# The taps' tile made 16 columns narrower: every tile allocated behind it moves down by 64 bytes

## The reference

```python
# 1: each head (8 heads of 24 channels) mixes 7 tokens with softmaxed taps, causal, zero-padded
w = softmax(weight, axis=-1)                      # weight: 8 x 7
out[b, s, h] = sum_k w[h, k] * x_pad[b, s + k, h]
# 2: a gated feed-forward, 192 -> 1536 -> 192
g = x @ w_gate;  x = (g * sigmoid(g) * (x @ w_val)) @ w_out
# 3: a second one with ELU, 192 -> 2048 -> 192
h = x @ w_in;  y = where(h > 0, h, exp(min(h, 0)) - 1) @ w_out2
```

## Time and profile before

| | us |
|---|---|
| median of 3 runs | 1193.2 (1192.63 to 1193.23) |
| the profiled execution's own time | 1191.55 |
| its span, first to last instruction | 1189.7 |
| PE busy | 1184.1 (100%) |
| PEld busy | 1051.1 (88%) |
| DVE, ACT, POOL busy | 772.7, 664.6, 699.6 |

### The profile page before, as it was taken

The page is one execution under the profiler, slowest core; times in us unless marked ns, Lnnn a source line. Parts: engine busy times, 40 slices in busy tenths (PEclk is TensorE's granted clock), DMA queues, the critical chain, the costliest instruction groups (busy, mean ns, idle before and its releaser), DMA issues.

```text
span 1189.7 us, 31406 instructions
## 1 busy us (share of the span) xinstructions
PE 1184.1 (100%) x11804; PEld 1051.1 (88%) x11804; DVE 772.7 (65%) x1192; ACT 664.6 (56%) x1113; POOL 699.6 (59%) x517
## 2 busy tenths in 40 slices
PE   9999999999999999999999999999999999999998
PEld 8889889898898988989888898888989889898898
DVE  7877565675656766566665766647667475675665
ACT  6557455464654646546465564655646555465564
POOL 6378565474654746547465474654756556475565
PEclk9999999999999999999999999999999999999999
DMA  8512011121101211012110021100212002120110
GB/s 179 121 43 45 18 31 32 31 44 31 24 20 31 44 31 26 18 31 44 31 35 17 22 44 31 35 18 22 44 31 44 9 22 44 31 44 9 32 33 15
DMA packets 103957, 43.38 MB, mean 36 GB/s; under 512 B 75889, under 2 KB 93937, under 8 KB 103921
## 3 DMA queue, kind: packets, MB, share of 16 engines
q1 hardware_dynamic: 103104, 42.29, 16.5%
q10 hardware_dynamic: 816, 0.59, 0.2%
HBM read 16.12 MB, written 6.29 MB: 19 GB/s over the span
## 4 chain that ended last, share of the span: by engine, by line
PE 97%; DVE 2%; issue 1%; ACT 0%; DMA 0%; SPq 0%; DVEq 0%; ACTq 0%
PE up L897 54%; PE down L897 42%; DVE hid_lo L740 1%; DVE mixed L702 1%; DVE hidden L759 0%; DMA in_b_lo<-in_b_lo 0%; DVE x_t L720 0%; DVE in_b_lo L708 0%; ACT act L568 0%; PE down L1108 0%; ACT out_w L324 0%; ACT hidden L641 0%; ACT in_b_hi L526 0%; ACT in_a_hi L646 0%; SPq L370 0%
## 5 line engine op out<-in xcount | busy, mean ns | idle before, releaser
L448 POOL TENSOR_TENSOR hid_lo<-hidden,hid_hi 128x512 fp32r<-128x512 f32 x435 | 607.1, 1407 | 464.6 <-ACT hid_hi L585 302.2
L897 PE MATMUL down<-out_w,hid_hi 64*128 64x384 f32 x2040 | 300.8, 355 | 0.0
L759 DVE TENSOR_TENSOR hidden<-act,up 128x512 f32<-128x512 f32 x191 | 131.0, 686 | 242.4 <-ACT act L568 242.4
L897 PE MATMUL down<-out_w,hid_lo 64*128 64x192 f32 x2040 | 263.0, 247 | 0.0
L800 DVE TENSOR_SCALAR act<-up 128x512 f32<-128x512 f32 x256 | 164.8, 686 | 107.5 <-PE up L897 105.4
L897 PE MATMUL up<-in_b_hi,up_w_hi 64*128 64x512 f32 x1128 | 226.1, 391 | 0.2 <-DMA in_b_lo<-in_b_lo 0.2
L897 PE MATMUL up<-in_b_lo,up_w_hi 64*128 64x512 f32 x1128 | 225.2, 389 | 0.0
L897 PE MATMUL up<-in_b_hi,up_w_lo 64*128 64x512 f32 x1128 | 224.5, 388 | 0.0
L585 ACT ACTIVATE hid_hi<-hidden 128x512 fp32r<-128x512 f32 x192 | 121.5, 633 | 174.9 <-DVE hidden L759 156.5
L621 ACT ACTIVATE hid_hi<-hidden 128x512 fp32r<-128x512 f32 x256 | 156.7, 628 | 96.8 <-DVE hidden L816 79.9
L897 PEld LDWEIGHTS down<-out_w,hid_lo 64*128 64x128 f32 x2040 | 202.1, 187 | 4.5
(11 more groups left out here) (99 smaller groups left out, 1100.6 us busy)
## 6 DMA issues: line engine op xcount, KB each, us to landing
x_raw<-x_dram SPq DMA_DIRECT2D x136, 64.0 KB, 2.3
out_dram<-stage SPq DMA_DIRECT2D x15, 384.0 KB, 2.7
in_b_hi<-in_b_hi SPq DMA_DIRECT2D x32, 128.0 KB, 2.3
in_b_lo<-in_b_lo SPq DMA_DIRECT2D x32, 128.0 KB, 2.3
swapped<-halves SPq DMA_DIRECT2D x32, 128.0 KB, 2.3
in_a_hi<-in_a_hi SPq DMA_DIRECT2D x30, 128.0 KB, 2.3
in_a_lo<-in_a_lo SPq DMA_DIRECT2D x30, 128.0 KB, 2.3
stage<-w_out_dram SPq DMA_DIRECT2D x7, 384.0 KB, 4.4
```

The costliest lines, as they stand in the source:

```text
L448: return pool.tensor_tensor(hid_lo[:, slot, :], hidden[:, s, :], hid_hi[:, slot, :].bitcast(F32), ALU.subtract)
L759: v.tensor_tensor(hidden[:, f % 2, :], act[:, f % 2, :], val_bank(f, n)[:, :], ALU.mult)\
L897: return nc.tensor.matmul(dst, lhsT, rhs, start=start, stop=stop, skip_group_check=True)
```

## The change

One constant, `WIDE`, goes from 120 to 104.

```diff
@@ mix_ffn_ffn
     WARM_BEFORE, WARM_AFTER = 6, 2
     PAIRS = (TAPS + 1) // 2
-    WIDE = 120
+    WIDE = 104
     assert N1 % RING == 0 and N2 % RING == 0 and 2 * TAIL == P and PER_BATCH == 8 and CHUNKS == 16
```

## The result

The changed kernel takes **1182.1 us** (median of 5 runs, 1180.6 to 1182.9) against 1193.2 (5 runs): ratio 0.9906, 95% interval 0.9893 to 0.992. It is faster by 11 us. The forecast was no change, in a range of 1187 to 1210, so both the forecast and the range were wrong.

A forecast was written before the change was run, and what follows sets the result against it. PE was taken as the bound, pair count times distance. Only the taps term counted, all others 0: 1191.55 - 0.1 = 1191.45 us for the profiled execution, 1193.2 - 0.1 = 1193.1 us against the median, range 1187 to 1210.

The forecast's parts named there:

- What bounds the kernel: In the chunks nobody makes PE wait; time is the number of matmul pairs times their distance, 228.8 ns for 512 columns.
- The columns, and what is on top of them: A 512- or 384-column pair costs its columns, 213 or 160 ns, plus about 15.5 ns.
- the 15.5 ns on top: Part of a 512-column pair's 228.8 ns beyond its columns, the only part a place in memory can change.
- The 192-column pairs: In down2_pair, each truly costs some 0.11 us, the length of one weight load, and delays its follower.
- the debt: About 0.025 us each 192-column pair hands on, because its follower's weights are not loaded when it has streamed.
- The taps matmuls, -0.1 us: At the start, 16 of 120 columns less in two fp32 matmuls saves between nothing and 0.14 us; taken as -0.1.
- DVE, ACT, POOL and DMA, 0: Their tiles move from 192 to 128 modulo 256; no effect, bounded by 0.5 us for engines, 0.2 us for DMA.
- The operands' places, 0: Moving and loaded operands all at 128 modulo 256 cost 4856 pairs nothing, nor 1016 that run on their load.
- case 3: Last project pair ahead of a down2_pair, moving tile and loading weights both at 192: 0.23 us, indistinguishable from other pairs.
- Case 4: Last 192-column pair of a down2_pair, moving tile and loading weights both at 128: 0.34 us with follower, as elsewhere.
- The faster rival: Reads in the same place run together, so 15.5 ns falls towards 3: 1132 us at full effect; chance 0.18.
- The slower rival: Equal places make a shared resource worse: values from 1196 to 1222 us, most below 1210; chance 0.24.

The follow-up runs named there:

- number 1: Changed kernel plus 64 unused bytes behind the taps' tile, putting all later tiles back at 192 modulo 256: 1193.0 us, ratio 1.0006.
- number 2: Changed kernel with the taps' tile 120 columns wide again and 192 unused bytes behind it, later tiles at 128 modulo 256: 1181.6 us, ratio 0.9904.
- number 3: Changed kernel plus 64 unused bytes ahead of the first weights, so weights and moving tiles all lie at 192 modulo 256: 1181.5 us, ratio 0.9908.
- experiment 8: Changed kernel with all tiles that TensorE does not read in the chunks put back to 192 modulo 256: 1182.4 us, ratio 0.991.
- Experiment 12: Changed kernel with only up1_w_lo and up2_w_lo at 192 modulo 256, everything else at 128: 1198.2 us, ratio 1.0041.
- number 7: Changed kernel with only hid_hi and hid_lo put back to 192 modulo 256: 1191.7 us, ratio 0.9986.
- experiment 16: Changed kernel with both operands of project at 192 modulo 256 and both of down1 and down2_pair at 128: 1191.9 us, ratio 0.9994.
- number 6: Changed kernel with only in_a and in_b put back to 192 modulo 256: 1194.9 us, ratio 1.0014.
- numbers 4: Changed kernel plus 128 unused bytes behind the taps' tile, weights at 128 and later tiles at 0 modulo 256: 1204.5 us, ratio 1.0095.
- 10: Changed kernel plus 32 unused bytes behind the taps' tile, a difference of 32 between moving tiles and weights: 1206.6 us, ratio 1.012.
- 11: Changed kernel plus 224 unused bytes behind the taps' tile, a difference of -32, or 224 around 256: 1205.7 us, ratio 1.0112.

## Why the prediction was wrong

**What bounds the kernel**: right. The time is the number of pairs times their distance, the other engines have slack, and 10.4 of the 10.8 us between the first `project` and the end were in that distance.

**The columns, and what is on top of them**: shown as far as the argument used it. By the starts, the first 384-column pair of a block takes 175.8 ns in the kernel before (109 of them), and (228.8 - 175.8) / 128 = 0.414 ns a column. That is what the prediction calls the 2.4 GHz level: 2.4 columns a nanosecond. The plain fp32 matmuls ahead of the chunks take twice that. Those of 128 columns (L1108) stand 0.76 / 7 = 0.109 us apart, those of 256 columns 0.216, and 0.107 us for 128 columns is 0.83 ns a column:

```profile
5.13 0.93 PE L1108 MATMUL down<-ident,stage 128*128 128x128 f32 x7
...
5.89 0.28 PE L897 MATMUL up<-ident 128*128 128x128 f32 x1
```

In the changed kernel that first 384-column pair is at 170.9 ns, which would give 0.436 ns a column. It is a border pair, so the 213.3 ns for 512 columns, and with them the 15.5 ns on top, remain estimates. In the long stretches with one difference the mean lay 13.4 to 20.0 ns above 213.3.

**The 192-column pairs**: the reading agrees with the starts of the loads, though no run tests it. The loads of weights in the kernel before, at the end of the same block:

```profile
611.10 0.20 PEld L897 LDWEIGHTS down<-out_w,hid_lo 64*128 64x128 f32 x2
611.28 0.19 PEld L897 LDWEIGHTS up<-in_a_hi,up_w_hi 64*128 64x128 f32 x2
611.39 0.20 PEld L897 LDWEIGHTS up<-in_a_hi,up_w_lo 64*128 64x128 f32 x2
```

The load for the follower starts at 611.28, with the 192-column pair, and the follower starts at 611.36, 88 ns later. The next load starts at 611.39: by the starts 108 ns behind the one before (892 of them in this trace), and 23 ns behind the start of its pair, where in a stream of 512-column pairs it is 3. The later 384-column pairs are at 199.2 ns, so the debt is 0.023 us, and 108 ns is the least distance of two pairs' loads in the chunks, the 0.11 us that the prediction took for the length of one. That length remains an estimate: the record of such a load is 184 ns long, in a stream of 512-column pairs too.

**The taps matmuls, -0.1 us**: not shown. Layouts with either width differ by less than the runs scatter (experiments 1 and 2). In the profile after, DVE got the taps 0.13 us later, not earlier, which does not follow the width: the transposes behind these matmuls began at 4.96 us in the traces of the kernel before (120 columns) and number 3 (104), and at 5.09 and 5.12 in those of number 1 (104) and number 2 (120). The next line answers to the earlier trace rows:

```profile
5.26 0.15 DVE L848 COPY tap_pairs<-down 64x4 f32<-64x4 f32 x1 [1.47 <-PE down L897]
```

**DVE, ACT, POOL and DMA, 0**: right for the time, by experiment 8, and by experiment 3, where their tiles all lie at 192 and the time is among the best. That DVE's own work would stay the same was not quite right: it was busy for 757.6 us in place of 772.7, most of it in the subtractions into `in_b_lo` (L708, 756 ns in place of 1202). PE waits for none of it, and number 8 has 775.4 us of DVE at the same time of the kernel.

**The operands' places, 0**: this is the step that failed, and it was case 3 in particular: the last pair of `project`, with `in_a_lo` moving from 192 while `hid_hi` loaded from 192, was taken for a pair of the changed kernel. The places were worth 2.2 ns on each of 3840 pairs and 2 ns on each of 1016 double steps. Three things were wrong with case 3.

- It took the place of the weights that load beside a pair for the one that counts. Experiment 12 puts most of the price behind the pair that uses the displaced weights, and number 7 none behind the pair beside whose run they load. By its own weights, at 128, that last pair was an ordinary pair of the kernel before. But its own operands don't settle its cost either.
- A single pair on a border says little about a run of equal ones, since a pair's distance depends on those ahead of it (12, 16). By the starts, this very pair takes 230.8 ns in the kernel before and 226.3 in number 6, with the same two places of its own operands, and 226.7 in the changed kernel. Case 4 was such a border too, and there the load set the pace and not the moving read, as the prediction itself read the 192-column pairs: their two loads are 108 ns apart, and their own distance is 88.
- Its resolution was 10 ns, while 0.5 ns a pair decided. The prediction said so, and still put 0.58 on no change.

**The faster rival** had the right sign: pairs with both operands at one place are the least costly, 226.7 ns. That reads in one place run together is not shown, and its size was off. It set 12.5 ns a pair as the full price, from the fp32 matmuls of the earlier trace rows, with the remark that a small part might come: 0.5 to 1 ns. It was 2.1 to 2.2 ns. Even in the best layout a pair keeps an estimated 226.7 - 213.3 = 13.4 ns over its columns. Its chance was 0.18, and the range, which ended at 1187, left out two thirds of it (0.12 of the 0.18).

**The slower rival** expected equal places to cost more. No run shows the price that its values up to 1222 us need, 6 ns a pair (29 us / 4856), nor that a shared resource is made worse by equal places, which was the author's estimate. The runs showed 2.1 to 2.2 ns a pair less with equal places, and unequal ones cost 11 us (64) or 22 to 25 us (32, 128, 192, 224) over the best.

The places of the two operands set the distance of pairs together. It is 226.7 ns with both at 128 and with both at 192 (number 3), and moving either side alone costs time: `in_a` and `in_b` 13 us (number 6), a part of the weights 16 us (number 12). Whether it is the reads that meet is not shown.

**What stays open**: by what mechanism the two places act on each other; why 32 costs as much as 192 and 64 so much less; where the rounds of two, three, four and seven pairs come from; and what the state is that pairs hand on to those behind them. No run here tells a conflict of the two reads from another coupling of load and matmul.

## What to carry to other kernels

Where TensorE is the bound and its matmuls come in a dense stream, try to allocate everything that it reads, weights and moving tiles alike, at one and the same place modulo 256 bytes (shown here for fp32r pairs of 64 rows whose slices start at multiples of 512 bytes in their tiles); a tile of a few columns in the wrong spot shifts all that follows, and was worth 1% here, 2% between the best and the worst layout. Move all of it or nothing: one set of tiles at the right place and another beside it lay between 0.14% under the kernel before (number 7) and 0.4% over it (number 12). And don't conclude from a border pair, at the timeline's resolution, on a price that thousands of pairs pay; a run of 50 or more gives the distance to 0.2 ns.

## What the runs showed of the hardware that was not expected

- The distance of two fp32r pairs (64 rows each, 512 columns, new weights for each, the clock granted in full) depends on the operands' places modulo 256 bytes: 226.7 ns for a difference of 0, 228.9 for 64, 232.3 for 128, and 233.3 for 32, 192 and 224.
- With one difference for all pairs, the distances still go in a fixed round: of three pairs for 64 (226, 229, 232 ns), of seven for 128, four for 32, two for 224 (the kernel before, numbers 4, 10 and 11).
- It has a memory: behind a step of place, pairs with equal places are slower by some 4 to 5 ns, four of them at the entry of `down1` and nine in the `project` behind it (experiment 16), and 16 pairs of a `down2_pair` in experiment 12 do not come back to the changed kernel's distance.
- Two pairs of 384 and 192 columns take 284 to 287 ns in all layouts but number 12 (290), and the pair behind a 192-column one is 0.02 to 0.03 us late in every one. From the start of the load beside a 192-column pair to the start of the next load it is 108.3 ns, also in every layout (887 to 899 of them in each trace).
- The time between the starts of a pair's two matmuls is a state too: about 25 ns early in the kernel before, 17 from 50 us and 10 from 100 us on, with a mean of 228.7 to 228.9 ns from pair to pair whichever it is. In the changed kernel it goes from 23 to 3 ns at 50 us, with 226.7 in both. It does not set the distance.
